# The second expert's tokens fetched as 128 rows from its first slot, all others one turn later, and its first weights issued ahead of the scatter's end

## The reference, cut to what matters

```python
logits = x @ w_gate
expert_idx = np.argmax(logits, axis=1)
...
for i in range(N):
    e = expert_idx[i]
    if counts[e] < capacity:
        disp[e, counts[e]] = x[i]
...
h = np.maximum(np.einsum('ecd,edf->ecf', disp, w1), 0.0)
y = np.einsum('ecf,efd->ecd', h, w2)
```

## Time and profile before

| | us |
|---|---|
| median of 3 runs | 396.7 (396.29 to 397.35) |
| profiled execution, its own time | 397.59 |
| its span in the trace | 395.8 |
| TensorE busy in it | 384.1 (97%) |
| ScalarE, VectorE, GpSimd busy | 235.2, 281.6, 116.1 |

### The profile page before, as it was taken

The page is one execution under the profiler, slowest core; times in us unless marked ns, Lnnn a source line. Parts: engine busy times, 40 slices in busy tenths (PEclk is TensorE's granted clock), DMA queues, the critical chain, the costliest instruction groups (busy, mean ns, idle before and its releaser), DMA issues.

```text
span 395.8 us, 6807 instructions
## 1 busy us (share of the span) xinstructions
PE 384.1 (97%) x2384; PEld 348.2 (88%) x2386; DVE 281.6 (71%) x446; ACT 235.2 (59%) x454; POOL 116.1 (29%) x122
## 2 busy tenths in 40 slices
PE   8999999999999998899999999999999999999994
PEld 3688999999999897899998999899899988999883
DVE  4888998899998644430447744569899998876851
ACT  6969879869887544430444654467666665444631
POOL 1853543643810250039999400000000000000014
PEclk9999999999999999899999999999999999999999
DMA  8684934974903347896798889090000000000004
GB/s 284 227 200 106 268 82 131 291 152 111 417 34 146 127 159 292 332 368 238 263 365 286 296 333 357 0 317 5 0 2 0 2 0 2 1 0 2 0 4 162
DMA packets 16124, 62.93 MB, mean 159 GB/s; under 512 B 3008, under 2 KB 3904, under 8 KB 11488
## 3 DMA queue, kind: packets, MB, share of 16 engines
q1 hardware_dynamic: 14560, 58.61, 43.9%
q0 software_dynamic: 1024, 3.22, 2.2%
q10 hardware_dynamic: 512, 0.73, 0.5%
HBM read 49.89 MB, written 3.22 MB: 134 GB/s over the span
## 4 chain that ended last, share of the span: by engine, by line
PE 58%; DMA 3%; POOL 1%; issue 0%; SPq 0%; POOLq 0%; ACT 0%; DVE 0%; ACTq 0%
PE ps L1088 17%; PE ps L1113 16%; PE ps L959 13%; PE ps L1006 8%; DMA ring<-in_w 2%; PE ps L1027 2%; DMA rows<-xg,sloti 1%; PE ps L987 1%; POOL rows L665 0%; SPq L520 0%; POOLq L102 0%; POOL out L687 0%; DVE outs L1751 0%; ACT yh L1320 0%; ACT ysb L1314 0%
## 5 line engine op out<-in xcount | busy, mean ns | idle before, releaser
L959 PE MATMUL ps<-xs,ring 128*128 x512 | 61.9, 280 | 2.4 <-DMA ring<-in_w 2.4
L959 PEld LDWEIGHTS ps<-xs,ring 128*128 128x128 f32 x512 | 60.8, 195 | 3.1 <-issue 2.7
L1555 DVE TENSOR_TENSOR ptl<-ps,pth 128x384 fp32r<-128x384 f32 x96 | 49.0, 552 | 4.3 <-ACT pth L1246 3.7
L1246 ACT ACTIVATE pth<-ps 128x384 fp32r<-128x384 f32 x96 | 41.9, 491 | 16.0 <-PE ps L881 15.7
L1478 DVE TENSOR_REDUCE nmax<-ps 128x1 f32<-128x768 f32 x48 | 45.7, 955 | 4.9 <-PE ps L751 2.0
L683 POOL DMA_INDIRECT spare<-fold,toki x1 | 1.0, 1009 | 161.4 <-PE ps L1113 161.4
L751 PE MATMUL ps<-ops 128*128 128x384 f32 x192 | 44.4, 353 | 0.8 <-DMA ops<-qo 0.7
L1200 ACT ACTIVATE prob<-ps,nmax 128x768 f32<-128x768 f32 x48 | 43.5, 906 | 0.2 <-DVE nmax L1478 0.2
L1088 PE MATMUL ps<-yh,wih 128*128 128x384 f32 x128 | 43.0, 336 | 0.3 <-ACT yh L1320 0.3
L1088 PE MATMUL ps<-yh,wlow 128*128 128x384 f32 x128 | 42.8, 335 | 0.0
L1088 PE MATMUL ps<-yl,wih 128*128 128x384 f32 x128 | 41.9, 335 | 0.0
(11 more groups left out here) (192 smaller groups left out, 782.9 us busy)
## 6 DMA issues: line engine op xcount, KB each, us to landing
ring<-in_w SPq DMA_DIRECT2D x32, 1024.0 KB, 4.8
wraw<-in_w_in SPq DMA_DIRECT2D x2, 1280.0 KB, 8.1
wraw<-in_w_out SPq DMA_DIRECT2D x2, 1280.0 KB, 10.8
ops<-kh SPq DMA_DIRECT2D x12, 192.0 KB, 6.0
ops<-qh SPq DMA_DIRECT2D x6, 384.0 KB, 8.2
xg<-rows SPq DMA_DIRECT2D x3, 513.0 KB, 4.9
raw<-in_vt SPq DMA_DIRECT2D x4, 384.0 KB, 5.3
wraw<-in_w_in SPq DMA_DIRECT2D x6, 256.0 KB, 4.4
```

Source lines behind the costliest of these rows:

```text
L959: last = mm(ps[:, fc // 2, (fc % 2) * WIDE:(fc % 2) * WIDE + W], wa[:, 2 * fc // KF, kd, P * (fc % (KF // 2)):P * (fc % (KF // 2)) + P], x ...
L1246: av(pth[:, (n // HT) % 2, HT * b:HT * b + HT, n % HT, :], ps[:, tile_banks(n)[b], 0:HALF].rearrange("p (a c) -> p a c", c=P), ACT.Copy).t ...
L1555: V.tensor_tensor(ptl[:, m2, HT * b:HT * b + HT, u, :], ps[:, tile_banks(n)[b], 0:HALF].rearrange("p (a c) -> p a c", c=P), pth[:, m2, HT ...
```

## The change

Five edits go together.

1. SP issues the second expert's first half of w1 (`first_weights(1, 0)`) when `Hw` is 2, and only then waits for the scatter's end.
2. After the scatter's end SP reads only 128 rows, from the second expert's first slot on, into the tile `second` (it lies over `hot`), with an address from a register. The slot is a new value `second_at`, made by one VectorE operation and loaded into a register by SP, ScalarE and VectorE.
3. The three DMAs of 513 KB (all rows) are issued behind the second expert's four halves of weights.
4. Between turns 0 and 1 TensorE makes 4 transposes (`second_rows`) in place of 24, and then waits for VectorE's copy (`xd`). Between turns 1 and 2 it makes the 24 (`all_rows`) and waits for part of the copies.
5. The first layer is written in parts (`layer_part`): fc = 0 and 1 with the first two blocks of features, then `turn_rows`, then their last two blocks, then the rest. The banks of the first product with `hot` change (`GATHER`).

```diff
+            V.tensor_scalar(second_at[:, :], ps[:, 2, 1:2], float(T - P), None, ALU.min).then_inc(s["bnd"], 1)
...
+            sp.wait_ge(s["bnd"], 2)
+            at_second = load_second(sp)
+            hold(sp, s["passed_sp"], s["Hw"], 2)
+            first_weights(1, 0)
             sp.wait_ge(s["sc"], 16 * NT)
             sp.wait_ge(s["perm"], KD)
-            for g in range(0, NT, NEAR):
+            sp.dma_start(second, rows[bass.ds(at_second, P), 0:DM]).then_inc(s["back"], 16)
+
+            def sorted_rows(g):
+
                 sp.dma_start(xg[:, g:g + NEAR, :], rows[P * g:P * g + P * NEAR, :].rearrange(
-                    "(p t) x -> p t x", t=NEAR)).then_inc(s["back" if g < FIRST_ROWS else "back2"], 16)
+                    "(p t) x -> p t x", t=NEAR)).then_inc(s["back2"], 16)
...
             for i in range(E - 1):
                 for half in range(2):
-                    hold(sp, s["passed_sp"], s["Hw"], 4 * i + 2 * half + 2)
-                    first_weights(i + 1, half)
+                    if i or half:
+                        hold(sp, s["passed_sp"], s["Hw"], 4 * i + 2 * half + 2)
+                        first_weights(i + 1, half)
                 for half, (read, many) in enumerate((("Yc", i + 1), ("w2l", 4 * i + 4))):
                     hold(sp, s["passed_sp"], s[read], many)
                     second_weights(i + 1, half)
+                if i == 0:
+                    for g in range(0, NT, NEAR):
+                        sorted_rows(g)
...
+                    pe.wait_ge(s["wa0"], 16 * (e + 1))
+                    pe.wait_ge(s["xa"], e + 1)
+                    pe.wait_ge(s["xd"], e + 1)
+                    layer_part(W, range(2), range(KD // 2))
...
+                        turn_rows(e + 1)
+                    pe.wait_ge(s["xa"], TURN * e + 2)
+                    pe.wait_ge(s["xd"], TURN * e + 2)
+                    layer_part(W, range(2), range(KD // 2, KD))
+                    layer_part(W, range(2, KF // 2), range(KD))
+                    pe.wait_ge(s["wa1"], 16 * (e + 1))
+                    layer_part(W, range(KF // 2, KF), range(KD))
...
+                def second_rows(s_done):
+
+                    for kd in range(KD):
+                        last = mm(ps[:, SLOW + 2 * kd // KD, P * (kd % 2):P * (kd % 2) + P], second[:, P * kd:P * kd + P],
+                                  c32("ident"), is_transpose=True, start=True, stop=True)
+                        if kd % 2:
+                            last.then_inc(s_done, 1)
+
+                def all_rows(s_done):
+
+                    pe.wait_ge(s["back2"], 16 * NT // NEAR)
+                    for b in REST_BANKS:
...
-                with pe.If(e < 1):
-                    rows_in()
+                with pe.If(e < 2):
+                    with pe.If(e < 1):
+                        pe.wait_ge(s["back"], 16)
+                        second_rows(s["xt"])
+                        pe.wait_ge(s["xd"], TURN + 2)
+                    with pe.Else():
+                        all_rows(s["xt"])
+                        pe.wait_ge(s["xa"], TURN + 3)
+                        pe.wait_ge(s["xd"], TURN + 3)
...
+                def second_rows():
+
+                    dve.wait_ge(s["xt"], 1)
+                    V.tensor_copy(xs[:, 0:KD // 2, bass.ds(at_second, P)], second_tiles(SLOW)).then_inc(s["xd"], TURN)
```

More of the change, by code:

```diff
@@ L139, in attention_moe_mish @@
         bounds = place("bounds", [P, E + 1, 2], I32)
-        mark = place("mark", [P, 5], F32)
+        second_at = place("second_at", [P, 1], I32)
+        mark = place("mark", [P, 3], F32)
         toki = place("toki", [P, NT], U32)
@@ L194, in attention_moe_mish @@
         hot = place("hot", [P, NT, NARROW], F32)
+        second = hot[:, 0:KD, :].rearrange("p t c -> p (t c)")
         xg = place("xg", [P, NT, DM + 1], F32)
@@ L326, in wait_task_read, with load_second @@
                 e.wait_ge(s["pa"], PA * (g - 1) + t - 4 + 1)
+        def load_second(engine):
+            return nc.values_load_multi_w_load_instructions(
+                second_at[0:1, 0:1], engines=(engine.engine,), min_val=0, max_val=T - P,
+                skip_runtime_bounds_check_because="at most T - P by the minimum that is written there")[1][0]
         def load_bounds(engine, e):
@@ L1048, in _ @@
             with nc.body("pe_more", parent=turn, valid_engines=[pe.engine]):
-                with pe.If(e < 1):
-                    pe.wait_ge(s["xa"], 3)
-                    pe.wait_ge(s["xd"], 3)
-                    pe.wait_ge(s["back"], 16 * FIRST_ROWS // NEAR)
-                    for kd in range(KD):
-                        for t in range(NEAR):
-                            at = WIDE * (kd % 2) + SHORT * t
-                            last = mm(ps[:, 4 + kd // 2, at:at + SHORT], xg[0:SHORT, t, P * kd:P * kd + P],
-                                      c32("ident")[0:SHORT, 0:SHORT], is_transpose=True, start=True, stop=True)
-                    last.then_inc(s["wide"], 1)
-                    pe.wait_ge(s["xw0"], 1)
-                    pe.wait_ge(s["xw1"], 1)
+                with pe.If(e < 2):
+                    with pe.If(e < 1):
+                        pe.wait_ge(s["xa"], 2)
+                        pe.wait_ge(s["wide"], 16)
+                        for kd in range(KD):
+                            last = mm(ps[:, SLOW, P * kd:P * kd + P], xg[:, 0, P * kd:P * kd + P], c32("ident"),
+                                      is_transpose=True, start=True, stop=True)
+                        last.then_inc(s["xwt"], 1)
+                        pe.wait_ge(s["wider"], 1)
+                    with pe.Else():
+                        turn_rows(e + 1)
+                        pe.wait_ge(s["xa"], TURN + 2)
+                        all_rows(s["xr"])
+                        pe.wait_ge(s["xra"], 1)
+                        pe.wait_ge(s["xrd"], 1)
                 pe.br_cond(n_e < MIDDLE + 1, "pe_middle", "pe_wide")
@@ L1292, in _, with all_rows @@
                 st, n_e = load_bounds(act, e)
-                def rows_in():
-                    for n, b in enumerate(XT_BANKS[0::2]):
-                        act.wait_ge(s["xt"], 2 * n + 1)
-                        av(many_slots(b), many_tiles(b), ACT.Copy).then_inc(
-                            s["xa"], 1 if b < SLOW else TURN * (E - 2) + 2)
+                def second_rows():
+                    act.wait_ge(s["xt"], 2)
+                    av(xs[:, KD // 2:KD, bass.ds(at_second, P)], second_tiles(SLOW + 1), ACT.Copy).then_inc(s["xa"], TURN)
+                def all_rows(s_ready, ready, s_part, s_all, many):
+                    for n, b in enumerate(REST_BANKS[1::2]):
+                        act.wait_ge(s_ready, ready + 2 * n + 2)
+                        done = av(many_slots(b), many_tiles(b), ACT.Copy)
+                        if n == 0 and s_part is not None:
+                            done.then_inc(s_part, 1)
+                        if n == 2:
+                            done.then_inc(s_all, many)
+                def rows_in():
+                    with act.If(e < 2):
+                        with act.If(e < 1):
+                            second_rows()
+                        with act.Else():
+                            all_rows(s["xt"], 2, s["xa"], s["xa"], ALL_TURNS - TURN - 3)
                 def narrow():
```

129 lines of the change are left out of this document (66 added, 63 removed).

## The result

The changed kernel takes 399.66 us (median of 6 runs, 399.48 to 400.84), the kernel before beside it 396.6 (6 runs, 396.29 to 397.35): ratio 1.008, 95% interval 1.0062 to 1.0098. It is 3.1 us slower; the prediction said 2.3 us faster. The profiled execution took 399.7 us with a span of 397.8.

What follows compares the result with a forecast made beforehand. TensorE, busy 97% of the span, was taken as the bound. Terms 0.47 + 1.3 + 12.96 + 2.60 + 0.5 + 0.1 = 17.93 against 20.24 us, 2.3 less, gave a median of 394.4 us, range 393.7 to 396.2.

Steps and rivals of the forecast that it cites:

- The wait for the first half of `w1`: Before turn 1: issued at 145.4, the half lands at about 150.2, so TensorE's 2.44 us wait goes.
- The wait for VectorE's copy: Between turns 0 and 1, new: 1.3 us idle (bounds 0.9 and 1.8), turn 1 starting 1.77 after turn 0's end.
- 24 transposes behind turn 1: Between turns 1 and 2: 2.60 us of transposes plus 0.5 idle (bounds 0 and 0.7); turn 2 may start at 3.07.
- The clock: Turn 1 keeps full clock; rival: it falls all the same, turn 1 costs 14.59, total 396.0 us, chance 0.13.
- the row I followed: Earlier profile before turn 1: clock at 1.00 through 2.40 us idle, 0.50 soon behind; a gap half as long keeps 2.4 GHz.
- Turn 0: First layer in parts: same products; last feature blocks wanted later can give 0.1 us, but nothing was counted.
- The base: Turn 0's end to turn 2's start took 20.24 us in one execution, itself 0.9 above the 396.7 median.
- Turn 1 12.96: Turn 1 at full clock takes 12.96 us, as turn 3 does, instead of 14.59.
- The register step: Before turn 0: operation about 0.2 us, cold load 1.15; block 1's copy ends at 140.6, with 0.5 us cover.
- The data rival: The 128 rows or w2's first half come late, TensorE waits about 1 us: 395.4 us, chance 0.11.
- The wait for w2's first half: In turn 1: smallest slack, 1.8 us; w2's first split waiting for its DMA would show the prediction wrong.
- The slower rival: Before turn 1: the early megabyte holds up the scatter, the 128 rows land late: 398.0 us, chance 0.05.

Runs made afterwards that it cites:

- r_early: The kernel before with only the second expert's first half of w1 issued early, ahead of the scatter wait: 395.12 us, ratio 0.9984 (0.9966 to 1.0002).
- x_head_late: x_head with the second expert's first half of w1 issued behind the scatter and the 128 rows: 394.84 us, ratio 0.9956.
- c_const: e1_head without registers, the 128 rows always read from and copied to slot 128 (for timing alone): 393.96 us, ratio 0.9948.
- x_head: e1_head a third time, unchanged, on the chip of x_before and x_after: 394.57 us, ratio 0.9948.
- x_after: The changed kernel once more, unchanged, on the chip of x_before: 397.65 us, ratio 1.0055.
- d_after128: The changed kernel with TensorE's code placed 128 bytes past a multiple of 256, nothing else: 397.37 us, ratio 1.0049.
- e2_order: The changed kernel with the first layer in its old order: 399.64 us, ratio 1.0096.
- e3_late: The changed kernel with the early half of w1 back behind the scatter and the 128 rows: 400.11 us, ratio 1.010.
- e4_bank: The changed kernel with the product with hot back in its old PSUM banks: 400.08 us, ratio 1.0117.
- c_align: e1_head with TensorE's code placed 128 bytes past a multiple of 256: 394.34 us, ratio 0.9951.
- d_again: e1_head once more, unchanged, in a later group: 394.56 us, ratio 0.9976.
- d_head64: e1_head with TensorE's code shifted by 64 bytes (HEAD = 64): 394.49 us, ratio 0.9981.
- y_align: c_align again, on another chip: 394.77 us, ratio 0.9963.
- first group: The runs e1_head, e2_order, e3_late and e4_bank, variants of the changed kernel on one chip: 396.5, 399.64, 400.11 and 400.08 us.
- second and the third group: Runs on what makes turn 0 long (r_regs, c_const, c_align, r_early), then on kernel or load (d_again, d_after128, d_head64, d_before128): ratios 0.9948 to 1.0049.
- e1_head: The changed kernel with TensorE's waits for copies moved from the branches at a turn's end to the next turn's head: 396.5 us, ratio 1.0018.
- x_before: The kernel before, unchanged, profiled again on the chip of x_after and x_head: 395.52 us, ratio 0.9987.
- d_before128: The kernel before with TensorE's code placed 128 bytes past a multiple of 256, nothing else: 394.02 us, ratio 0.9975.
- r_regs: The kernel before with only second_at written and loaded into registers, used by nobody: 396.21 us, ratio 1.0004.

## Why the prediction was wrong, point by point

**The wait for the first half of `w1`: gone, as said.** It was 2.4 us in the profile of before and isn't in any profile of the change. Only, it takes one edit and not both: r_early has the early half and all the rows, x_head_late the 128 rows and the half behind them, and neither waits for `ring` before turn 1.

**The wait for VectorE's copy (1.3 of idle, bounds 0.9 and 1.8): this term failed.** It came out as 2.15 of idle, in a gap of 2.74 instead of 1.77. The copy starts 1.10 behind the first transpose's load, not 0.48. Of these 0.62, 0.24 come from the load: in the row of before the transposes followed idle time and product and load began together, while here the load runs ahead of its product, behind the last one of turn 0 (0.72 in c_const with the same four transposes, where load and first product begin at 153.47 and 153.70). The other 0.38 is the copy's address from a register, which c_const hasn't; the prediction had 0.05 for it. The copy takes 0.42, as worked out from the earlier trace rows. Then come the branches and the start: 1.21 against the 0.6 for three branches and 0.22 for a start, so 0.4 more. The earlier trace rows gave the right price of one branch (174 to 209 ns in four of the rows above), but not of the register steps and the spaces between them, which come to as much again. x_head shows the price of the whole path by taking it away: 0.98 of 1.21.

**24 transposes behind turn 1 (3.07, and 0.1 for the branch in turn 2): 4.30.** VectorE's second copy ends 2.43 behind turn 1's end, for which I had 2.25. The way from there to the first load is 1.87, for which I had 0.82, the same three branches and start as at turn 1. But turn 2 is a wide one: it goes through `pe_more`, with a branch in it (L1087) and one behind it (L1102), five in all (L1079 stands here for L1075). With 0.2 of copy and 1.05 of path this is the largest mistake. The blocks could have been counted in the code. In x_head the whole step costs 2.74, since the branches run while the transposes do.

**The clock.** In the first profile of after it stayed at 1.00, as forecast. But it is a chance and not a yes or no. In x_after and d_after128, 7 of 20 executions have a mean granted clock of 0.994 or 0.995 and take 398.99 to 400.39; the other 13 have 0.998 or more and take 396.83 to 397.74. The idle stretch there is 2.15 to 2.19 us. In the earlier runs with such a stretch (the changed kernel, e2_order, e3_late, e4_bank) 6 of 19 have 0.994 or 0.995. In the six runs with 1.17 us of idle in its place (c_align, d_again, d_head64, x_head, x_head_late, y_align) none of 54 executions has less than 0.997, and none takes more than 395.98. So the rival was right in a third of the executions, at some 2 us each, since the gap was longer than on paper. That the length of the stretch decides is likely but not shown for itself, since the repaired kernels lack the idle time ahead of turn 2 as well. The Trainium skill's rule that the prediction weighed (TensorE: Matmul & The Clock Gate, What's actually happening) holds in so far as one length of idle time met both levels; that a gap half as long kept 2.4 GHz agrees with the row I followed.

**Turn 0 (12.9, "I count nothing"): failed in the profile of after, and not by the change's own work alone.** It was 14.38 there, and 14.3 to 14.4 with late signals in the first group, but 12.93 to 12.96 in all nine later profiles of changed kernels, among them identical copies of both kinds (x_after, d_again and x_head). That c_const and c_align seemed to cure it was the chip or the load: both my theories of the second and the third group (registers, place of the code) fell with d_again. It may be the change and a circumstance together, since the runs of before in the first group stood at 395.73, no higher than elsewhere; but this isn't shown, as before wasn't profiled there. What the circumstance is, stays open. Its price is the difference of e1_head and d_again: 1.4 us in turn 0, and 1.0018 against 0.9976. So of the 5.3 us between forecast and result 2.1 are the two gaps, whose cause is shown, 1.4 turn 0 and 0.8 its start, whose causes aren't, and 1.0 the execution of before from which I counted.

**The base.** The sum was made against 20.24 us of one execution. Other profiles of the same program between the same points have 19.31 (x_before), 17.51 and 18.04 (both with `HEAD = 128`): the wait for the rows or for `ring`, and the clock behind it, come and go. I took off 0.9 for the whole execution, but counted the gain of the stretch from its worst case. And the 12.96 of turn 3 was no measure for turn 1 of before, though I took it for a confirmation: at full clock that turn takes 13.38 to 13.50, as it waits for w2 (x_before). So the low clock cost it 1.1 to 1.2, not 1.63, and with 128 rows ahead of w2 in place of 1.5 MB the change takes about 0.4 off that turn at full clock, by another way than I said. Against 17.5 the repaired change has 17.54 (x_head: 153.99 to 171.53), nothing won. The transposes show why: before needs 2.77 for 24 and 1.37 idle (d_before128), 4.14; x_head needs 0.58, 1.17 and 2.74, 4.49, and its turn 1 is 13.05 against 13.38. The change pays for four more transposes and a second place where TensorE waits for copies, and takes back only what late data and the clock cost.

**The other terms.** Turn 1 12.96: measured 12.95. The register step: writing and loading it is free, as said (r_regs); its use in the copy's address is not (above). The data rival: TensorE never waits for the half or for the 128 rows, though in the first profile they landed 8.0 and 5.3 us after issue, the rows at 156.1, 0.2 before they were wanted. The wait for w2's first half that I named as a sign does come in x_head and x_head_late, on ScalarE, and costs turn 1 only 0.1 to 0.2. The slower rival: its mechanism is there, since the early megabyte holds up the scatter's count by some 1.1 us (x_head against x_head_late, one profile each), but the rows still came in time. The kernel came out slower by the gaps and by turn 0.

## What to carry to other kernels

A wait placed in front of branches costs their whole path too, here 1.2 us through three and 1.9 through five; put it at the head of the next block, and only for what that block reads first. An address from a register in the copy that is waited for is on the path as well, here 0.4 us. Before a stall in one profiled execution is counted as a gain, see whether it is in other executions: here the spread of before's runs (394 to 398 us) was as large as the stall. And an idle stretch of TensorE is priced with the clock behind it, as a chance.

## What was not expected of the hardware

TensorE's results reached ScalarE and SP late in turn 0, by 2.85 us at the first (4.05 instead of 1.20 behind the 56 loads), while its own rows were evenly spaced and the granted clock was 1.00 (the stretch 141.88 to 156.26 above). It was there in the first five profiles of changed kernels, and in none of the nine after, with identical kernels on both sides (the changed kernel and x_after, e1_head and d_again). It cost 1.4 us. The cause is open.

A shift of TensorE's code by 128 bytes made the kernel before 0.3% faster twice (0.9975 and 0.9965) and drew its runs together (1.3 and 1.6 us wide against 3.7 to 3.8 beside them); on the repaired change no effect is seen: a shift by 64 changes nothing on one chip (d_again 0.9976, d_head64 0.9981), and a shift by 128 (c_align 0.9951, y_align 0.9963) lies between the unshifted d_again and x_head (0.9948), each on another chip. The profiles show that the half of `w1` was issued 0.6 to 1.1 us earlier (149.84 and 149.35 against 150.44, with a start of turn 0 only 0.15 to 0.28 earlier), as SP's first read came 3.8 and 4.2 us behind the last scatter's start and not 4.6, and that the clock didn't fall. One more thing differs in the traces. Between 134 and 160 us the queue `q8 instruction` moves one block at 135 to 137 and one at 148 to 159 in every profile with the code unshifted, and only one, at 142 to 145, in every shifted one. Whether that is the cause, no run shows.
